# A fused attention and two feed-forward layers on one core: the first tiles of v by row and by TensorE, squares in pairs of rows, the split rows a piece later

## The reference

```python
qn = q / (np.linalg.norm(q, axis=1, keepdims=True) + 1e-06)
kn = k / (np.linalg.norm(k, axis=1, keepdims=True) + 1e-06)
s = kn.transpose(0, 2, 1) @ qn / tau          # 256 x 256
a = softmax(s)
x = v @ a                                     # 6016 x 256
xn = x / rms(x) * rms_g
x = (silu(xn @ w_gate) * (xn @ w_val)) @ w_out      # 256 -> 1536 -> 256
h = x @ w_in                                        # 256 -> 2048
out = (h - tanh(h)) @ w_out2                        # 2048 -> 256
```

## Time and profile before

| | before |
|---|---|
| median of 3 runs | 1206.84 us (1206.53 to 1208.21) |
| the profiled execution | 1209.15 us |
| its span, first to last instruction | 1207.2 us |
| TensorE (PE) busy | 1185.5 us |
| VectorE (DVE) busy | 847.7 us |
| ScalarE (ACT) busy | 366.4 us |
| GpSimd (POOL) busy | 33.9 us |
| mean granted clock of TensorE | 0.994 |

### The profile page before, as it was taken

How to read it: one execution, slowest core, us unless ns; L and a number is a source line. 1 busy time by engine, 2 the same in 40 slices (tenths; PEclk the granted TensorE clock), 3 DMA queues, 4 the chain that set the end, 5 groups by cost and what they waited for, 6 DMA issues and landing times.

```text
span 1207.2 us, 15962 instructions
## 1 busy us (share of the span) xinstructions
PE 1185.5 (98%) x5348; PEld 990.7 (82%) x5348; DVE 847.7 (70%) x1363; ACT 366.4 (30%) x585; POOL 33.9 (3%) x29
## 2 busy tenths in 40 slices
PE   7889999999999999999999999999999999999998
PEld 6768788888888888888888888888888888888998
DVE  4787767668686586586676766767868658658665
ACT  5664731321231232231141142132223123123121
POOL 4510000000000000000000000000000000000000
PEclk9989999999999999999999999999999999999999
DMA  8624201002002001001101100200200100100100
GB/s 279 217 71 122 70 6 30 1 1 35 0 0 35 0 0 29 6 0 17 17 0 17 17 0 1 33 0 0 35 0 0 30 0 0 18 1 1 18 1 14
DMA packets 112314, 33.92 MB, mean 28 GB/s; under 512 B 100768, under 2 KB 108192, under 8 KB 112288
## 3 DMA queue, kind: packets, MB, share of 16 engines
q1 hardware_dynamic: 111856, 33.05, 11.3%
q10 hardware_dynamic: 432, 0.52, 0.1%
HBM read 27.40 MB, written 6.16 MB: 28 GB/s over the span
## 4 chain that ended last, share of the span: by engine, by line
PE 94%; DMA 1%; DVE 1%; POOL 1%; issue 1%; ACT 0%; SPq 0%; DVEq 0%; ACTq 0%; POOLq 0%
PE ring L909 53%; PE out_acc L922 21%; PE y_acc L922 16%; PE out_acc L880 2%; DMA qk_in<-in_q_dram 1%; PE y_acc L847 1%; POOL qk_lo L379 1%; PE y_acc L856 1%; PE out_acc L866 0%; PE ring L985 0%; PE y_acc L893 0%; SPq L311 0%; POOL vt_lo L372 0%; ACT qk_hi L438 0%; PE y_acc L880 0%
## 5 line engine op out<-in xcount | busy, mean ns | idle before, releaser
L475 ACT ACTIVATE act<-ring 128x512 f32<-128x512 f32 (+1 forms) x333 | 196.5, 590 | 721.9 <-PE ring L909 705.3
L722 DVE TENSOR_TENSOR h_lo<-act,h_hi 128x512 fp32r<-128x512 f32 (+1 forms) x336 | 228.7, 681 | 10.7
L718 DVE TENSOR_TENSOR act<-ring,act 128x512 f32<-128x512 f32 (+1 forms) x192 | 129.3, 674 | 98.5 <-ACT act L475 98.3
L709 DVE TENSOR_TENSOR act<-ring,act 128x512 f32<-128x512 f32 (+1 forms) x141 | 95.0, 674 | 145.9 <-ACT act L475 145.9
L909 PE MATMUL ring<-x_hi,wl_hi 128*128 128x512 f32 (+1 forms) x384 | 148.8, 387 | 3.3 <-DVE wl_lo L575 3.3
L909 PE MATMUL ring<-y_hi,wl_hi 128*128 128x512 f32 (+1 forms) x384 | 148.9, 388 | 1.7 <-DVE y_lo L729 1.7
L909 PE MATMUL ring<-x_lo,wl_hi 128*128 128x512 f32 (+1 forms) x384 | 148.6, 387 | 0.0
L909 PE MATMUL ring<-x_hi,wl_lo 128*128 128x512 f32 (+1 forms) x384 | 148.6, 387 | 0.0
L909 PE MATMUL ring<-y_hi,wl_lo 128*128 128x512 f32 (+1 forms) x384 | 147.8, 385 | 0.0
L922 PE MATMUL out_acc<-h_hi,wl_hi 128*128 128x512 f32 (+1 forms) x384 | 147.8, 385 | 0.0
L909 PE MATMUL ring<-y_lo,wl_hi 128*128 128x512 f32 (+1 forms) x384 | 147.7, 385 | 0.0
(11 more groups left out here) (154 smaller groups left out, 1604.7 us busy)
## 6 DMA issues: line engine op xcount, KB each, us to landing
v_in<-in_v_dram SPq DMA_DIRECT2D x88, 64.0 KB, 2.2
out_dram<-out_rows SPq DMA_DIRECT2D x88, 64.0 KB, 1.8
qk_in<-in_k_dram SPq DMA_DIRECT2D x10, 512.0 KB, 6.7
qk_in<-in_q_dram SPq DMA_DIRECT2D x10, 512.0 KB, 7.8
w_in<-in_moe_w_out_dram SPq DMA_DIRECT2D x14, 256.0 KB, 2.9
w_in<-in_moe_w_in_dram SPq DMA_DIRECT2D x8, 256.0 KB, 3.1
w_in<-in_moe_w_gate_dram SPq DMA_DIRECT2D x6, 256.0 KB, 2.8
w_in<-in_moe_w_val_dram SPq DMA_DIRECT2D x6, 256.0 KB, 3.2
```

The costliest lines, as they stand in the source:

```text
L475: nc.scalar.activation(act[:, u % RING, 0:width], bank(name)[:, 0:width], func).then_inc(act_ready, 1)
L709: nc.vector.tensor_tensor(buf, bank(gate)[:, 0:width], buf, ALU.mult).then_inc(bank_free, 1)
L718: nc.vector.tensor_tensor(buf, bank(hidden)[:, 0:width], buf, ALU.subtract).then_inc(bank_free, 1)
L722: nc.vector.tensor_tensor(h_lo[:, u % RING, 0:width], act[:, u % RING, 0:width], f32(h_hi[:, u % RING, 0:width]), ALU.subtract).then_inc(h ...
```

## The change

Four parts, all in the code before tile 1.

1. Tiles 0 and 1 of v are loaded whole, one DMA of 512 KB each in runs of 1 KB, behind pieces 4 and 5. TensorE turns them, half a tile at a time (four 128x128 transposes, `turn_first`), ahead of pieces 7, 8, 9 and 10, into two banks of `ring`. ScalarE casts a half from PSUM behind the squares of pieces 8 to 11, and VectorE subtracts behind the sums of pieces 9 to 12. The third turn waits until the first bank has been read by VectorE, the fourth for the second bank.
2. Squares are added into two rows instead of four (to leave the two banks), so a wide piece takes two additions of half the size. `PIECES` ends in 2, 2, 2, 1 and not in 4, 2, 1. At the last piece but one three additions of 128x512 give one row for the norms; there are two `add_norms` in place of five, and no `tensor_reduce`.
3. The split rows of a piece are multiplied a piece later, behind the whole rows of the next one. A split piece counts as used only then. Split pieces are 3 to 10, one fewer.
4. The first three weight blocks, now ("gv", 0), ("gv", 1), ("gv", 2), are loaded behind pieces 6, 7 and 8, cast on ScalarE behind pieces 9, 10 and 11, and split by GpSimd behind its last piece. ("down", 0) is the fourth early block, split by VectorE after the softmax. The other blocks come one unit earlier or so in tile 0. In the loop, SP loads v two tiles ahead, after the store.

```diff
-PIECES = (1, 1, 2, 4, 4, 4, 4, 4, 4, 4, 4, 4, 4, 2, 1)
+PIECES = (1, 1, 2, 4, 4, 4, 4, 4, 4, 4, 4, 4, 2, 2, 2, 1)
...
-EARLY = 3
+EARLY = 4
...
+V_LOAD = (4, 5)
+W_LOAD = (6, 7, 8)
+V_TURN, V_CAST, V_SPLIT = 7, 8, 9
+W_CAST = (9, 10, 11)
...
-WARM_NORMS = ((3, 0, 512, 128),)
-WARM_SOFTMAX = ((3, 4, 0, 128), (3, 12, 0, 128), (3, 4, 4, 128))
+WARM_NORMS = ((4, 0, 512, 64),)
+WARM_SOFTMAX = ((3, 4, 0, 128), (3, 12, 0, 128), (5, 4, 4, 128))
...
-    blocks = [("gv", 0), ("gv", 1), ("down", 0), ("gv", 2), ("gv", 3), ("down", 1), ("gv", 4), ("gv", 5), ("down", 2)]
+    blocks = [("gv", 0), ("gv", 1), ("gv", 2), ("down", 0), ("gv", 3), ("down", 1), ("gv", 4), ("gv", 5), ("down", 2)]
...
-    LATE = {u: EARLY + n for n, u in enumerate((1, 3, 4, 5, 6, 7, 8, 9, 10, 11, G + 1, G + 3, G + 5, G + 7))}
+    LATE = {u: EARLY + n for n, u in enumerate((2, 3, 4, 5, 6, 7, 8, 9, 10, 11, G + 1, G + 3, G + 5))}
...
+                if i in V_LOAD:
+                    t = V_LOAD.index(i)
+                    sp.dma_start(v_first[:, t, :, :], v_rows[t * TILE:(t + 1) * TILE, :].rearrange(
+                        "(g p) c -> p g c", p=P)).then_inc(v_loaded_first, 16)
+                if i in W_LOAD:
+                    load_block(W_LOAD.index(i))
...
                 if i >= SLOTS:
-                    act_e.wait_ge(sq_added, i - SLOTS + 1)
+                    act_e.wait_ge(sq_added, added[i - SLOTS + 1])
                 nc.scalar.activation(qk_sq[:, i % SLOTS, :, 0:n, :], qk_in[:, stage, :, 0:n, :],
                                      ACT.Square).then_inc(squares_ready, 1)
-                if i - 3 in V_PIECE:
-                    cast_v(V_PIECE.index(i - 3), TILE)
+                if V_CAST <= i < V_CAST + 2 * KC:
+                    n = i - V_CAST
+                    act_e.wait_ge(v_turned_first, n + 1)
+                    nc.scalar.copy((vt_hi, vt1_hi)[n // KC][:, n % KC, :], turn_bank[n % 2]).then_inc(v_hi_first, 1)
+                if i in W_CAST:
+                    split_block(W_CAST.index(i))
...
+                if i < PAIR:
+                    nc.vector.tensor_copy(sq_acc[:, :, i, :], sq[:, :, 0, :]).then_inc(sq_added, 1)
+                elif i < COUNT - 2:
+                    for h in range(PIECES[i] // PAIR):
+                        dve.wait_ge(sq_added, added[i] + h)
+                        nc.vector.tensor_tensor(sq_acc[:, :, :, :], sq_acc[:, :, :, :],
+                                                sq[:, :, h * PAIR:(h + 1) * PAIR, :], ALU.add).then_inc(sq_added, 1)
...
-                if i - 2 in V_PIECE:
-                    turn_v(V_PIECE.index(i - 2), TILE)
+                if V_SPLIT <= i < V_SPLIT + 2 * KC:
+                    n = i - V_SPLIT
+                    dve.wait_ge(v_hi_first, n + 1)
+                    nc.vector.tensor_tensor((vt_lo, vt1_lo)[n // KC][:, n % KC, :], turn_bank[n % 2],
+                                            f32((vt_hi, vt1_hi)[n // KC][:, n % KC, :]),
+                                            ALU.subtract).then_inc(v_first_ready, 1)
...
+            def piece(i):
+
+                if i in split_at:
+                    whole_rows(i)
+                    if i - 1 in split_at:
+                        split_rows(i - 1).then_inc(qk_used, 1)
+                else:
+                    if i - 1 in split_at:
+                        split_rows(i - 1).then_inc(qk_used, 1)
+                    whole_rows(i).then_inc(qk_used, 1)
+
+            def turn_first(n):
+                t, c = n // KC, n % KC
+                if c == 0:
+                    pe.wait_ge(v_loaded_first, 16 * (t + 1))
+                if n >= 2:
+                    pe.wait_ge(v_first_ready, n - 1)
+                for g in range(TILE // P):
+                    ins = nc.tensor.transpose(turn_bank[n % 2][:, g * P:(g + 1) * P],
+                                              v_first[:, t, g, c * P:(c + 1) * P], ident[:, :])
+                ins.then_inc(v_turned_first, 1)
...
-            for i in range(COUNT - 2):
+            for i in range(COUNT - 1):
+                if i == V_TURN:
+                    pe.wait_ge(constants, IDENT)
+                if V_TURN <= i < V_TURN + 2 * KC:
+                    turn_first(i - V_TURN)
                 piece(i)
```

More of the change, by code:

```diff
@@ L63, in build @@
     assert PER_P * P == N and sum(PIECES) == PER_P and sum(PIECES[:FIRST_WIDE]) == WIDE
-    assert all(n == WIDE for n in PIECES[FIRST_WIDE:COUNT - 2]) and PIECES[COUNT - 2:] == (2, 1)
+    assert all((n == WIDE) == (FIRST_WIDE <= i <= LAST_WIDE) for i, n in enumerate(PIECES))
+    assert PIECES[:FIRST_WIDE] == (1, 1, 2) and PIECES[COUNT - 2:] == (2, 1)
     piece_at = [sum(PIECES[:i]) for i in range(COUNT)]
-    split_at = list(range(FIRST_WIDE, COUNT - 2 - WHOLE))
+    split_at = list(range(FIRST_WIDE, LAST_WIDE))
+    added = [0]
+    for i in range(COUNT - 1):
+        added.append(added[-1] + (3 if i == COUNT - 2 else max(PIECES[i] // PAIR, 1)))
     BLOCK = 1024
@@ L173, in build @@
         first_sigmoid = vt
[L174 to L177, removed]
+        partial = act[:, 2, :].rearrange("p (w c) -> p w c", c=C)
+        totals = act[:, 0, :].rearrange("p (w c) -> p w c", c=C)
+        partial = act[:, 2, :].rearrange("p (w c) -> p w c", c=C)
         raw_rows = act[:, 1, :].rearrange("p (m c) -> p m c", m=KC)
@@ L402, in cast_v @@
             def cast_v(t, width):
[L403 to L406, removed]
+                act_e.wait_ge(v_turned, t - 1)
+                nc.scalar.copy(vt_hi[:, :, 0:width], vt[:, :, 0:width]).then_inc(vt_hi_ready, 1)
             def split_block(n):
@@ L559, in turn_v @@
             def turn_v(t, width):
[L561 to L564, removed]
+                dve.wait_ge(v_loaded, (t - 1) * TILE_DMAS)
+                nc.vector.transpose(vt[:, :, 0:width].rearrange("p k (b r) -> p k b r", r=SQ),
+                                    v_in[:, :, 0:width // SQ, :]).then_inc(v_turned, 1)
             def split_v(t, width):
-                dve.wait_ge(vt_hi_ready, t + 1)
+                dve.wait_ge(vt_hi_ready, t - 1)
                 nc.vector.tensor_tensor(vt_lo[:, :, 0:width], vt[:, :, 0:width], f32(vt_hi[:, :, 0:width]),
@@ L839, in _, with whole_rows @@
         def _(pe):
[L840 removed]
+            def whole_rows(i):
                 stage, n = i % STAGES, PIECES[i]
[L843 removed]
                 pe.wait_ge(qk_loaded[stage], 32 * (i // STAGES + 1))
[L845 removed]
+                for j in range(SPLIT_ROWS if i in split_at else 0, n):
                     for m in range(KC):
@@ L861, in piece, with split_rows @@
-                ins.then_inc(qk_used, 1)
+                return ins
+            def split_rows(i):
+                s = split_at.index(i)
+                pe.wait_ge(qk_split, s + 1)
+                for j in range(SPLIT_ROWS):
+                    for m in range(KC):
+                        for k_part, q_part in PASSES:
+                            ins = nc.tensor.matmul(raw[:, m, 0:C],
+                                                   (qk_hi if k_part else qk_lo)[:, s % SLOTS, 0, j, m * P:(m + 1) * P],
+                                                   (qk_hi if q_part else qk_lo)[:, s % SLOTS, 1, j, :],
+                                                   start=False, stop=False)
+                return ins
```

118 lines of the change are left out of this document (44 added, 74 removed).

## The result

The changed kernel takes 1211.91 us in the median of five runs (1211.14 to 1213.09), the kernel before 1206.84 in five beside it (1206.14 to 1208.21). The ratio is 1.0042 with a 95% interval of 1.0027 to 1.0057: slower by 5.1 us. The profiled execution of the changed kernel took 1211.14 us.

The account below looks back on a forecast made before the run. TensorE, busy 1185.5 of 1207.2 us, bounds the kernel, and the first 95 us decide the time. Terms of +11.2, -0.9 and -5.8 sum to +4.5 us on the median 1206.84: 1211.3 us, range 1204.5 to 1217.

Parts of the forecast that it names:

- The loads and the pace up to piece 8: Start: loads of pieces 5 to 9 come 4.03 us apart, piece 9 at 33.3; TensorE ends piece 8 at 32.5.
- The new wait: Ahead of the third and fourth turn, at pieces 9 and 10: TensorE waits 6.9 and 6.3 us for VectorE's subtraction.
- The turns: Four 128x128 transposes of half a tile of v on TensorE: 0.86 us per turn, lower bound 0.24.
- The falls of the clock: TensorE's clock falls at both waits for the subtraction of v, at pieces 9 and 10: 2.9 us added to each.
- term one: The start up to the norms: ready at 72.1 us instead of 60.9, +11.2 us.
- The softmax: Behind the norms: x waits for the softmax alone and begins sooner, -0.9 us (between 0 and -1.4).
- Tile 0: From the end of unit 3 to unit 5 of tile 0: 6.0 us instead of 11.8, -5.8 us.
- the case without waits: Rival, chance 0.04: TensorE goes on at 32.5 without waiting at pieces 9 and 10, norms at 53.1; -14.5 us, 1192.3 us.
- The rule of the Trainium skill that transposes don't count for the clock: Part of a rival, chance 0.19: at both late turns the clock returns 1.7 us later, 0.86 us more each, 1213.1 us.

Follow-up runs that it names:

- e1: The changed kernel with VectorE's subtraction of v moved ahead of the two additions of the same piece: 1199.99 us.
- e2: The changed kernel with the split rows multiplied in their own piece again, not a piece later: 1202.54 us.
- e5: The changed kernel with the subtraction of v ahead of its piece's additions, and the third and fourth turn, with their casts and subtractions, a piece later: 1196.42 us.
- e4: The changed kernel with 24 products that nobody reads ahead of each of the two waits for the subtraction of v: 1208.32 us.
- e7: The kernel before, unchanged, one more execution with its trace: 1206.67 us.
- e6: As e5, but with the split rows multiplied in their own piece: 1196.84 us.
- e8: The changed kernel, unchanged, one more execution with its trace: 1211.36 us.

## Why the prediction was right

The prediction was 1211.3 us, slower by 4.5; measured 1211.9, slower by 5.1. Its mechanism stood, term by term, but two errors of size met.

- **The loads and the pace up to piece 8.** Piece 9 was forecast for 33.3 and came at 33.4; piece 8 was to end at 32.5 and ended at 32.9. The forecast had 4.03 us from piece to piece; TensorE began pieces 7 and 8 at 25.46 and 29.50, 4.04 apart. (Before, there are ten wide pieces, 3 to 12, not eleven.)

- **The new wait.** Forecast 6.9 and 6.3 us, measured 6.65 and 6.12. e1, e2 and e5 take it apart. The second wait needs both the subtraction behind the additions and the count a piece late: it is gone with either undone. The first needs the turn so early: with the count on time it is 4.96 us (e2), with the subtraction first 2.69, for the additions of piece 8 (e1), and with the turn a piece later as well it is gone (e5).
- **The turns.** 0.86 us each was forecast, between 0.24 and 0.86 (a quarter of 0.86 is 0.22). The row of four transposes lasts 0.60 us, but the next product starts 0.44 us behind its start (37.33 and 37.77 in e5), so a turn holds TensorE for half of the forecast; the 1.1 us that the prediction gave beside it was further off.
- **The falls of the clock** were the term that was mis-sized: 2.9 us each, from one row of the trace, against 1.35 and 2.5 in the profiled execution (39.57 to 44.68 and 50.80 to 57.08, less the 3.76 that a turn and the products of a piece take at full clock, 37.33 to 41.09 in e5) and 3.6 together by e4. With 2.0 us less for the falls, 1.0 less for the two waits and the two turns with their pieces (3.76 us each, not 4.02), and with piece 8 through 0.4 later, term one was +8.8 us and not +11.2 (72.1 forecast for the norms, 69.7 measured). Why 2.9 was too much stands in the rows of the clock: the cost is half of the stretch that lies behind the wait. Before, 6.0 of the 6.8 us at half lay behind the wait of 3.33 us. The clock fell 2.5 us into the wait of 6.65 us and 4.4 us into that of 6.12, and was at half for 6.8 us again, so 4.1 and 1.7 us of it passed while TensorE stood still anyway.
- **The softmax.** 4.8 us from the norms to the first product of x, where it was 5.5: -0.7 for the forecast -0.9.
- **Tile 0.** -6.0 us between the profiled executions, for the forecast -5.8. Against an ordinary execution of before (e7: unit 4 to unit 5 in 93.20 - 86.16 = 7.0 us, and 3.3 of waiting) it is -4.7.

So the sum of the terms by the two profiled executions is 8.8 - 0.7 - 6.0 = +2.1 us, which is what these two differ by (1211.14 - 1209.15 = 2.0), and not the 5.1 of the medians. Against e7, whose norms were ready at 60.1, it is 9.6 - 0.7 - 4.7 = +4.2, and the executions differ by 4.5; the profiled execution of the changed kernel was the fastest of its five, 0.8 us under the median. The profiled execution of before had been an unlucky one, as its 2.3 us above the median said. I took that for an offset to be subtracted, while it was a part of the very terms that the change removes. That the forecast came within 0.6 us is luck: the falls behind the new waits were overrated by 2 us, and the gain where the old falls went by about as much (1.1 in tile 0, 0.8 at the norms).

Of the rivals, the case without waits is what e5 measured (14.5 us less than before was forecast, 10.5 measured). Its norms came at 54.7 us and not 53.1, and against e7 they are 5.4 us earlier, with 0.7 us won in the softmax and 4.7 in tile 0: 10.8. The rule of the Trainium skill that transposes don't count for the clock ("TensorE: Matmul & The Clock Gate", Part 4: PE-mode transpose) would have shown as stretches at half longer than the old 6.0 us by 1.7. Begun by a turn, they were 2.7 and 5.1, 5.2 in e2 and 6.1 in e1, and counted from the fall of the clock all four lasted the same 6.8 us as the old one, so no run here bears it out. As plain products follow each turn, none refutes it either.

## What to carry to other kernels

Before an edit is costed by durations, follow each new wait backwards through the queues of all engines, to see whether the chain it waits for can start before the waiting engine arrives: a semaphore that counts one step later may close a circle, and an edit that is worth nothing by itself can be dear beside another. The late count changes 0.4 us with the turns spaced (e5 and e6) and 9.4 with them as they were (e2 and the changed kernel); the place of turns and subtractions alone costs 5.7 us (e2 and e6). The mend here was not to take the change back: an instruction moved ahead of its neighbours, and the turns that waited one piece later, made of a loss of 5 us a gain of 10.5. And where a term of the sum rests on a fall of TensorE's clock, take its size from several executions, or give it as a range.

## What the runs showed of the hardware

A wait of 2.69 us was enough for the clock to fall (e1). The stretches at half behind a wait were 2.7 and 5.1 us long in the changed kernel, 2.9 and 5.2 in its second execution (e8), 3.2 (e7), 5.2 (e2), 6.0 (before) and 6.1 (e1), while the waits themselves repeat to 0.1 us. Counted from where the clock fell, each time within the wait, all of these lasted 6.8 us but the one of e7, which lasted 3.4. No run shows what decides between the two.

Four float32 transposes of 128x128 held TensorE for 0.44 us from the start of the first to the next product (e5), 0.11 us each, where half of a float32 product of 256 columns would be 0.22.

One small instruction of VectorE took 2.31 us in the changed kernel, and 0.22 before; it reads two elements per partition. In all other traces of the changed kernel and its variants it took 2.29 to 2.31, and the additions of piece 7 came some 0.6 us late, which cost nothing, as those of piece 8 waited for ScalarE in any case (0.99 us here, 1.13 in e1). In each of these traces it lies inside a subtraction of GpSimd and the two end within 0.03 us of each other (28.96 and 28.99 here), while GpSimd was idle when it took 0.22. So it looks as if it had waited for GpSimd; that the two contend is inferred, and no run separates it.

```profile
26.56 2.40 POOL L388 TENSOR_TENSOR qk_lo<-qk_in,qk_hi 128x1024 fp32r<-128x1024 f32 x1 [1.67 <-ACT qk_hi L442]
26.68 2.31 DVE L653 TENSOR_SCALAR tau<-tau,tau_c 128x2 f32<-128x2 f32 x1
```
